# Last stage of a long-convolution and MLP kernel: GpSimd makes the slope of pair q+1 in front of the den of pair q

## The reference

```
h = x @ w_in                      # 24960 tokens, 128 -> 2048
P = a[0] + a[1]*h + a[2]*h**2 + a[3]*h**3
Q = 1.0 + |b[0]|*|h| + |b[1]|*h**2
out = (P / (Q + 1e-6)) @ w_out    # 2048 -> 128
```

## Time and profile before

| | |
|---|---|
| median of 3 runs | 2175.2 us (2174.44 to 2179.35) |
| the profiled execution | 2174.0 us, span 2172.2 us |
| mean granted TensorE clock | 0.983 of full speed |
| first slope, last den (start) | 630.1 us, 2158.7 us |
| busy shares of the span | PE 92%, POOL 87%, DVE 84%, ACT 84% |

### The profile page before, as it was taken

How to read it: one execution, slowest core, us unless ns; L and a number is a source line. 1 busy time by engine, 2 the same in 40 slices (tenths; PEclk the granted TensorE clock), 3 DMA queues, 4 the chain that set the end, 5 groups by cost and what they waited for, 6 DMA issues and landing times. The chain is left out here.

```text
span 2172.2 us, 33906 instructions
## 1 busy us (share of the span) xinstructions
PE 2009.2 (92%) x8964; PEld 1463.6 (67%) x8964; DVE 1832.5 (84%) x2511; ACT 1824.1 (84%) x2671; POOL 1892.2 (87%) x1218
## 2 busy tenths in 40 slices
PE   7999499999959999999999999999999999999997
PEld 4777499999936666666666666666666666666664
DVE  4888488888849898989898988989888988898987
ACT  4888466666649998999999989999998989998998
POOL 3777398888839999999999999999999999999997
PEclk9999799999969999999999999999999999999999
DMA  6999766677531111111111111111111111111100
GB/s 178 312 305 309 191 162 172 178 181 180 128 86 31 31 31 31 30 31 30 31 30 31 34 31 31 30 33 50 36 31 31 30 31 30 31 30 31 30 13 12
DMA packets 65791, 175.60 MB, mean 81 GB/s; under 512 B 5046, under 2 KB 8414, under 8 KB 62686
## 3 DMA queue, kind: packets, MB, share of 16 engines
q1 hardware_dynamic: 65694, 174.67, 29.5%
HBM read 102.89 MB, written 71.76 MB: 80 GB/s over the span
## 5 line engine op out<-in xcount | busy, mean ns | idle before, releaser
L635 POOL TENSOR_TENSOR den<-slope,mag 128x832 f32<-128x832 f32 x480 | 948.1, 1975 | 43.4 <-POOL slope L627 4.6
L879 PE MATMUL acc_p<-g_s,w_out_k 128*128 128x416 f32 x1920 | 775.8, 527 | 61.3 <-DVE oT L801 38.5
L760 DVE SCALAR_TENSOR_TENSOR num<-square,level,h_p 128x832 f32<-128x832 f32 x480 | 517.7, 1078 | 116.2 <-ACT square L668 82.6
L627 POOL TENSOR_SCALAR slope<-mag,den_c 128x832 f32<-128x832 f32 x480 | 500.3, 1042 | 79.6 <-ACT mag L660 46.3
L879 PEld LDWEIGHTS acc_p<-g_s,w_out_k 128*128 128x128 f32 x1920 | 343.4, 190 | 315.5 <-issue 184.6
L793 DVE SCALAR_TENSOR_TENSOR g_s<-num,ratio,r_p 128x832 f32<-128x832 f32 x480 | 517.6, 1078 | 41.0 <-ACT r_p L684 26.8
L668 ACT ACTIVATE square<-h_p,centre 128x832 f32<-128x832 f32 x480 | 477.9, 996 | 7.7 <-DVE mag L755 5.3
L868 PE MATMUL h_p<-xy_hi,w_lo 128*128 128x416 f32 x960 | 448.5, 467 | 32.1 <-DVE num L760 29.5
L677 ACT ACTIVATE den<-den 128x832 f32<-128x832 f32 x480 | 450.1, 938 | 21.2 <-POOL den L635 21.1
L684 ACT ACTIVATE r_p<-den 128x832 f32<-128x832 f32 x480 | 436.2, 909 | 0.7 <-DVE g_s L793 0.7
L868 PE MATMUL h_p<-xy_lo,w_hi 128*128 128x416 f32 x960 | 338.0, 352 | 0.0
(11 more groups left out here) (79 smaller groups left out, 2807.9 us busy)
## 6 DMA issues: line engine op xcount, KB each, us to landing
bent<-bent_s SPq DMA_DIRECT2D x60, 576.0 KB, 6.2
bin_s<-bent SPq DMA_DIRECT2D x24, 1440.0 KB, 9.7
x_s<-in_x SPq DMA_DIRECT2D x60, 416.0 KB
back<-back_s SPq DMA_DIRECT2D x24, 960.0 KB, 7.8
vin_s<-back SPq DMA_DIRECT2D x30, 768.0 KB, 5.9
v_s<-in_v SPq DMA_DIRECT2D x30, 416.0 KB
out<-o_s SPq DMA_DIRECT2D x60, 208.0 KB
pos_s<-in_pos_emb SPq DMA_DIRECT2D x30, 88.0 KB
```

Source lines behind the costliest of these rows:

```text
L627: nc.gpsimd.tensor_scalar(slope[:, q % DEEP], mag[:, q % DEEP], den_c[:, 1:2], den_c[:, 0:1], ALU.mult, ALU.add).then_inc(slope_done, 1)
L635: nc.gpsimd.tensor_tensor(den[:, q % DEEP], slope[:, q % DEEP], mag[:, q % DEEP], ALU.mult).then_inc(den_done, 1)
L760: nc.vector.scalar_tensor_tensor(out=num[:, q % NUMS], in0=square[:, q % SQUARES], scalar=level[:], in1=h_p[:, q % 2, :, 0:TOK], op0=ALU.a ...
L879: mm = nc.tensor.matmul(acc_p[:, 0:TOK], w_out_k[:, ft], g_s[:, q % DEEP, t], start=(ft == 0), stop=(ft == FT - 1))
```

## The change

It is on GpSimd's queue alone, and in the order alone. Before: slope 0, den 0, slope 1, den 1, ... After: slope 0, then slope q+1 in front of den q for every q. The slope has four buffers before and after (`DEEP` = 4), and every instruction keeps its waits. The last turn is taken out of the loop and written out, since it has no slope behind its last pair; the loop has 13 turns in place of 14.

```diff
                 pool.wait_ge(coef_ready, 1)
+                slopes(0, 0)
                 for q in range(PER):
-                    slopes(0, q)
+                    slopes((q + 1) // PER, (q + 1) % PER)
                     dens(0, q)
-                with pool.Fori(1, ITERS) as i:
+                with pool.Fori(1, ITERS - 1) as i:
                     for q in range(PER):
-                        slopes(i, q)
+                        slopes(i + (q + 1) // PER, (q + 1) % PER)
                         dens(i, q)
+                for q in range(PER):
+                    if q + 1 < PER:
+                        slopes(ITERS - 1, q + 1)
+                    dens(ITERS - 1, q)
```

## The result

| | before | after |
|---|---|---|
| median | 2174.93 us (20 runs, 2171.81 to 2179.35) | 2180.91 us (20 runs, 2175.41 to 2184.80) |
| profiled execution | 2174.0 us, span 2172.2 | 2180.8 us, span 2179.0 |
| ratio to before | | 1.0024, 95% interval 1.0016 to 1.0031 |

The changed kernel is 0.24% slower, 5.2 us by the ratio (3.5 to 6.7). The direction and the mechanism were forecast; the size was forecast at 12.4 us.

The account below looks back on a forecast made before the run. The prediction took ACT with its own stalls as the bound, POOL following with play. Lost play cost 28 x 0.42 = 11.8 us plus 14 x 0.04 = 0.6, 12.4 us, giving 2187.6 us against 2175.2; range 2176 to 2206.

Parts of the forecast that it names:

- The bound: Last stage: ACT with its own stalls sets about 51 us a block; POOL follows it with play.
- Rival (a): GpSimd is the bound and its saved gap comes through: 53 us less, 2122 us; chance 0.07 with a milder form.
- Price 1: POOL: the gap before the den goes, 2.98 us a pair in place of 3.09; by itself worth nothing.
- Rival (c): The gap before the den stays, POOL's pair stays at 3.09 us: 42 us slower, 2217 us; chance 0.08.
- Price 2: The slope's new place: den q waits behind magnitude q+1, which cuts the play from 3.8 to 0.59 us.
- the play: Time by which a magnitude could come later before a logarithm waits for its den: 3.8 us before, 0.59 after.
- Price 3: What the lost play costs ACT, walked along the rows: 11.8 us plus 0.6, 12.4 us in all.
- short passages: Three steps between xy_hi copies, or from o_s at m=2 to the first: 0.51 us, under 0.59, cost nothing.
- long passage: From the second xy_hi copy (m=8) to the o_s copy (m=14): 0.42 us each, 28 times, 11.8 us.
- four-step passages: From o_s at m=14 to o_s at m=2: 0.04 us in every second block, 14 times, 0.6 us.
- They don't take up ACT's waiting: PE and DVE hang on ACT's output, so they give nothing of ACT's new waiting back.
- The tail: From slope 460 to the last den POOL sets the end, 61.6 us in both orders: nothing gained or lost.

Follow-up runs that it names:

- gap_only: Kernel before, order kept, den made as mag x mag so that it has no wait for its slope: 2173.82 us, ratio 0.9991.
- short_new: Changed order, slope over one of two tiles and den as mag x mag, against the kernel before: 2172.53 us, ratio 0.9989.
- x_old: Kernel before with the first xy_hi split and the second group each a step later, POOL's order kept: 2153.32 us, ratio 0.9898.
- lead5_new: Changed kernel with the magnitudes one pair further ahead (LEAD_E 5, LEAD_H 7): 2175.07 us, ratio 1.0000 to the kernel before.
- lead3_old: Kernel before with the magnitudes one pair less ahead (LEAD_E 3, LEAD_H 5): 2219.76 us, ratio 1.0199.
- part_order: Changed kernel, but pairs m=9 to 13 of each block keep the old order: 2174.70 us, ratio 0.9997 to the kernel before.
- after_2: The changed kernel again with no edit, for a second trace: 2184.07 us in one execution, 4 clock falls.
- after_3: The changed kernel again with no edit, for a third trace: 2188.32 us in one execution, 7 clock falls.
- x kernels: Kernels with xy_hi splits a step later, in old or changed order: 2151.68 to 2156.46 us; one with the second x product left at m=7: 2168.89 us.

## Why the prediction was wrong in size and right in kind

- **The bound** (first part): right. gap_only and short_new take 0.5 us and more a pair from POOL and move the kernel by 2 us, x_old takes a stall from ACT and gives 22. Rival (a), the gap's 53 us, is out. In the turn of the earlier trace rows POOL was busier than ACT and DVE, and it was the follower. Perfetto Trace Analysis in the Trainium skill ("Identifying the Most-Contended Engine") would have the engine of the highest occupancy optimized first; for this stage the runs speak against it. TensorE, busy for 96.11 us of that turn, is a rival that no experiment tested by itself. Against it stand its waits in the kernel before, from 690 to 2090 us: all are for DVE, 23.4 us for `num` and 11.1 us for `g_s` among them, which follow ACT's square and exponential. And in the steps of 2.81 us ACT alone is busy throughout. From logarithm 219 to 223 before (PE, PEld, DVE, ACT, POOL):

```profile
1335.51:1346.74 11.23, 10.96 (x40) 7.34 (x41) 10.58 (x13) 11.23 (x17) 10.82 (x8) 1.00 0.00 0
```

- **Price 1**, the gap goes: right, and a little more. A den starts 1.00 us after its slope, not 1.02, so that POOL's pair is 2.96 us, not 2.98. The pair lost 0.13 us (3.09 to 2.96), where the idle time listed in front of the dens had been 0.09. Rival (c), the gap that stays, is out.
- **Price 2**, the play: right. 0.24 us from the magnitude's end to slope 220 (1335.14 to 1335.38, with magnitude 220 at 1334.63 + 0.51) and 0.02 to 0.03 us from a den's end to its logarithm stand in the rows after as in those before. lead5_new gives one step of play back to the changed order, and the cost goes to nothing; lead3_old takes one from the order of before, which then costs 44 us.
- **Price 3**, the walk: the places are right, to the logarithm (221 to 223 in the example, then the o_s copy), and nothing at the short passages. **The step that failed is the size of this term, where I gave 28 x 0.42 + 14 x 0.04 = 12.4 us.** The long passage measured 0.34 to 0.35, since the deficit a step is 2.96 - 2.81 = 0.15 and not 0.17: 28 x 0.345 = 9.7 us. A cost that is the difference of two nearly equal paces shrank by a fifth on 0.02 us. The 14 x 0.04 of the four-step passages measured nothing.
- **"They don't take up ACT's waiting"** failed in part. This was the second step that failed, a term put at nothing: the step at m=17 of the turn (m=1 of its second block), in which ACT's square waits for DVE's magnitude, is 3.07 us in all three traces of the changed kernel against 3.17, and the loop's head is shorter by 0.04 to 0.07: 14 x 0.15 = 2.1 us back. The head's part is uncertain, as the head differs by 0.03 between traces of kernels without these waits; the 0.10 is clear. In lead5_new and part_order, where ACT doesn't wait before, it is 3.17 again. That PE and DVE catch up on their backlog in the waits is argued from this, not shown apart.
- **The tail**, costed at nothing, gave 0.6 us back: from logarithm 448 to 479 93.85 us before, 93.23 after (93.36 and 93.33 in after_2 and after_3).
- The sum with these sizes is 9.7 - 2.1 - 0.6 = 7.0 us, and the traces less their clock falls give 7 to 8. The timed runs say 5.2 (3.5 to 6.7) by the ratio, and 6.0 by the medians. What is left is 1 to 2 us, and the clock, which the prediction left out, can make it up. The falls in unprofiled executions aren't listed, but the mean granted clock of each execution is: 0.9836 in the mean of the 20 of the changed kernel, and 0.9826 in that of 58 executions of the kernel before, timed beside the experiments. A fall costs 1.7 us of full clock (0.44 + 1.00 + 0.24 in the windows of the last section), 0.0008 of the span. So the changed kernel had some 1.3 falls fewer, worth 1.8 us at 1.4 us each. This is an estimate: the mean clock takes in the first two stages too, and the 58 aren't the 20 of the ratio. The 20 themselves bear it out: the three at 0.981 took 2184.5 us in the mean, the two at 0.986 2176.1. With these 1.8 us the timed runs give 7 to 8 us, as the traces do. Why the changed kernel had fewer falls is open.
- The first trace alone would have misled on the size: between first and last logarithm it has only 4.3 us of difference, as it had 2 falls against 4. It also began its last stage 2.3 us later than the first trace of before (first slope at 632.43 and 630.12 us), but so do gap_only and part_order, with 633.4 and 632.3: that is not the change's.

## What to carry to other kernels

Before an engine's gap is filled, look at who waits for it. Here POOL was busy 94% of the turn and its results lay unused for 1 to 5 us: it was a follower, and work taken from it came back as waiting. A reordering on an in-order queue has a price in play even when every wait is covered today; write the loop out (which steps lie between the result that is now waited for and the one that is now held) and compare it with the places where the leader stalls. And count play in starts, from the timeline: ACT's waits of 0.15 us, no longer than the overlap of two of its instructions, stood in no list of waits. Last, a size that is a small difference of paces, times a count, needs the clock of the executions beside it: falls of the clock moved single executions here by as much as the change did.

## What the runs showed of the hardware that was not expected

**TensorE's clock falls at the head of some loop turns.** PE stands still there for 2.2 to 2.5 us in each of 12 turns, while ACT's loop starts anew. In some turns the granted clock goes from 2.4 to 1.2 GHz just after. From after_2, a row of PE's timeline, then the windows (the last three numbers of each are the granted clock, the DMA share and GB/s):

```profile
1361.71 1.82 PE L884 MATMUL acc_p<-g_s,w_out_k 128*128 128x416 f32 x4 [2.40 <-DVE oT L806]
```

```profile
1360.00:1364.00 4.00, 2.29 (x6) 1.52 (x7) 3.93 (x5) 3.83 (x6) 3.45 (x3) 0.89 0.01 2
1364.00:1366.00 2.00, 2.00 (x8) 1.79 (x8) 1.47 (x3) 1.81 (x3) 2.00 (x2) 0.50 0.00 0
1366.00:1368.00 2.00, 2.00 (x9) 1.36 (x8) 1.32 (x2) 1.41 (x3) 0.63 (x2) 0.88 0.00 0
1368.00:1370.00 2.00, 2.00 (x11) 1.52 (x9) 1.52 (x2) 2.00 (x4) 2.00 (x2) 1.00 0.52 125
```

The granted clock is 0.50, 1.2 GHz, from 1364 to 1366 us and back at 1.00 by 1368; a turn with a fall is 1.4 us longer (103.4 to 103.5 us before, against 101.9 to 102.2). The same idle time in the next turn may have none. There were 2 to 4 falls in the loop turns in every trace with the turn of before, 2, 4 and 7 in those of the changed kernel, 7 to 11 in those of lead3_old and the x kernels. What decides is open.

**GpSimd's product is shorter when both operands are one tile:** 1.574 us in gap_only and 1.575 in short_new against 1.976 for slope x mag in the changed kernel, same shape; none of the three has idle time in front of it.
